# Sliding-window attention in front of two gated feed-forward stages: scores of 64 queries of both heads as one block-diagonal product

## The reference

```
# attention: batch 4, 8 heads, 576 positions, head size 64
scores = q @ k.T / sqrt(64)
scores = where(0 <= i - j < 128, scores - slope[h] * |i - j|, -1e9)
attn   = softmax(scores)           # sum has 1e-9 added
x      = attn @ v                  # heads side by side: 2304 tokens x 512
# first feed-forward stage, inner size 1536
x = (sigmoid(x @ w_gate) * (x @ w_val)) @ w_out
# second stage, inner size 1024
x = ((x @ w1) * (x @ w2)) @ w3 @ w_out2
```

## Time and profile before

| what | us |
|---|---|
| median of 3 timed executions | 923.81 |
| profiled execution, its own time | 921.83 |
| its span | 920.0 |
| PE busy | 891.7 |
| POOL busy | 611.5 |
| DVE busy | 531.9 |
| ACT busy | 487.5 |

### The profile page before, as it was taken

One profiled execution on the slowest core, in us unless ns is written; L12 is line 12 of the kernel. 1 busy time (PEld: TensorE's weight loads), 2 busy tenths in 40 slices (PEclk: granted clock), 3 DMA queues, 4 the chain that ended last, 5 costly groups with the idle time before them and its releaser, 6 DMA issues.

```text
span 920.0 us, 15518 instructions
## 1 busy us (share of the span) xinstructions
PE 891.7 (97%) x5336; PEld 798.6 (87%) x5336; DVE 531.9 (58%) x1235; ACT 487.5 (53%) x1075; POOL 611.5 (66%) x502
## 2 busy tenths in 40 slices
PE   6999999999999999899999999999999999999998
PEld 4666888998988888788898888889999999999997
DVE  5555655565457545555555545755666555575554
ACT  6666585566645644657565654654344333345330
POOL 4449489667654886639956674597769977747930
PEclk9999999999999999999999999999999999999999
DMA  6554423222221222232321322203231221112201
GB/s 227 167 166 137 134 90 109 81 64 74 87 70 61 88 96 88 73 113 95 95 93 44 100 71 67 75 25 92 70 115 68 71 76 66 66 67 70 69 24 69
DMA packets 46142, 80.77 MB, mean 88 GB/s; under 512 B 4208, under 2 KB 27376, under 8 KB 46064
## 3 DMA queue, kind: packets, MB, share of 16 engines
q1 hardware_dynamic: 45648, 79.32, 26.7%
q10 hardware_dynamic: 416, 0.46, 0.1%
HBM read 72.94 MB, written 6.82 MB: 87 GB/s over the span
## 4 chain that ended last, share of the span: by engine, by line
PE 74%; POOL 7%; DVE 6%; issue 5%; ACT 5%; DMA 2%; SPq 0%; ACTq 0%; DVEq 0%; POOLq 0%
PE quad_ps L577 12%; PE quad_ps L579 11%; PE quad_ps L578 11%; PE o_ps L577 10%; PE o_ps L579 9%; PE o_ps L578 9%; PE attn_ps L631 4%; PE attn_ps L599 2%; POOL wo_lo L1223 2%; PE attn_ps L614 2%; PE quad_ps L614 1%; PE quad_ps L599 1%; POOL wq_lo L1210 1%; ACT soft L757 1%; DVE quad_ps L1015 1%
## 5 line engine op out<-in xcount | busy, mean ns | idle before, releaser
L577 PE MATMUL quad_ps<-xs_hi,wq_hi 128*128 128x384 f32 x840 | 292.7, 348 | 4.1 <-POOL wq_lo L1217 2.4
L579 PE MATMUL quad_ps<-xs_hi,wq_lo 128*128 128x384 f32 x840 | 281.6, 335 | 0.0
L578 PE MATMUL quad_ps<-xs_lo,wq_hi 128*128 128x384 f32 x840 | 281.2, 335 | 0.0
L577 PEld LDWEIGHTS quad_ps<-xs_hi,wq_hi 128*128 128x128 f32 x840 | 157.6, 188 | 23.5 <-issue 15.7
L577 PE MATMUL o_ps<-h_hi,wo_hi 128*128 128x384 f32 x480 | 167.1, 348 | 4.5 <-DVE xf L1031 2.3
L579 PE MATMUL o_ps<-h_hi,wo_lo 128*128 128x384 f32 x480 | 161.2, 336 | 0.0
L578 PE MATMUL o_ps<-h_lo,wo_hi 128*128 128x384 f32 x480 | 161.1, 336 | 0.0
L1173 POOL TENSOR_TENSOR soft<-soft,recip 128x512 f32<-128x512 f32 (+2 forms) x80 | 73.6, 920 | 130.6 <-DVE recip L933 130.3
L578 PEld LDWEIGHTS quad_ps<-xs_lo,wq_hi 128*128 128x128 f32 x840 | 157.9, 188 | 0.0
L579 PEld LDWEIGHTS quad_ps<-xs_hi,wq_lo 128*128 128x128 f32 x840 | 157.7, 188 | 0.0
L1210 POOL TENSOR_TENSOR wq_lo<-raw_q,wq_hi 128x768 fp32r<-128x768 f32 x60 | 110.6, 1843 | 68.9 <-ACT wq_hi L791 68.9
(11 more groups left out here) (62 smaller groups left out, 1371.9 us busy)
## 6 DMA issues: line engine op xcount, KB each, us to landing
raw_q<-w SPq DMA_DIRECT2D x24, 512.0 KB, 3.6
raw_q<-w_gate SPq DMA_DIRECT2D x18, 512.0 KB, 3.5
raw_q<-w_val SPq DMA_DIRECT2D x18, 512.0 KB, 4.4
wo_lo_raw<-w_out SPq DMA_DIRECT2D x18, 512.0 KB, 3.6
wo_lo_raw<-w_times_wout SPq DMA_DIRECT2D x12, 512.0 KB, 3.8
w_raw<-w3t SPq DMA_DIRECT2D x16, 256.0 KB, 3.0
outT<-xf SPq DMA_DIRECT2D x8, 384.0 KB, 4.3
q_sb<-qT SPq DMA_DIRECT2D x15, 192.0 KB, 3.9
```

The lines of the kernel that those rows point to most:

```text
L577: pe.matmul(out, lh, rh, start=start, stop=False, skip_group_check=onto)
L578: pe.matmul(out, lh, rl, start=False, stop=False, skip_group_check=onto)
L579: return pe.matmul(out, ll, rh, start=False, stop=stop, skip_group_check=onto)
```

## The change

It touches attention alone. A unit is now 64 queries of both heads. `q_sb` holds, for each unit, a block of 128 rows by 128 columns with the first head's queries in the upper left and the second head's in the lower right; the other two quarters are set to zero once, by six DVE memsets at the start, and the loads write only the blocks: two DMAs for each load of `q`, with pieces of 64 queries (256 bytes). A score matmul takes such a block as weights (128 rows) against all 128 rows of `k_sb`, and gives 128 rows (64 queries of one head above 64 of the other) by 192 keys. A full step has two units and two matmuls of 192 columns; a start step one of 64 and one of 128 columns; a half step one unit, one matmul of 192 columns. `score`, `exponentials` and `normalise` follow this: one instruction per unit of 128 rows by 192 columns (for normalise one for both units). A half step has two transposes instead of four, and `pv` runs over only the queries that are there. Both units' scores lie in one bank. In the head there are two such banks in turn, so `scores(n)` waits for DVE's reading of step n-2. Later `scores` and `pv` share `attn[0]` and `turn` has `attn[1]`: `turn` no longer waits for DVE's reading of the section's scores, `pv` does. In the head `q` and `k` have a third buffer, in memory that is unused until the first feed-forward product P4, and all loads of `q` and `k` are issued one job (in sections: one section) earlier. The bias is half as many rows and 192 columns (96 KB instead of 256 KB).

```diff
@@ sets, buffers
-QC, KC = 3 * P, 4 * P
+KC = 4 * P
+U = P // 2
+UW = WINDOW + U
+QC = 6 * P
...
 def set_of(j):
+    return j % 3 if j < HEAD_JOBS else j % 2
+def v_set(j):
     return j % 2
...
+def units_of(n):
+    return rows_of(n) // U
+def keys_from(n, u):
+    return P - u * U if starts_batch(n) else 0
...
+            q_2, k_2 = sb(early, "q_2", [P, QC // 2], F32), sb(early, "k_2", [P, KC // 2], F32)
...
+        def score_cols(n, u):
+            bank = quad[n % 2] if n < HEAD else attn[0]
+            return bank[:, u * UW + keys_from(n, u):(u + 1) * UW]
         def turn_bank(n):
-            return quad[2 + n % 2] if n < HEAD else attn[0]
-        def pv_bank(n):
-            return attn[n % 2] if n < HEAD else attn[1]
+            return quad[2 + n % 2] if n < HEAD else attn[1]
+        def pv_cols(n):
+            return attn[n % 2][:, 0:rows_of(n)] if n < HEAD else attn[0][:, 2 * UW:2 * UW + rows_of(n)]
+        def q_units(st, h, of, units):
+            return q_sb[st][h * U:(h + 1) * U, 0:units * P].rearrange("p (u h n) -> p u h n", h=2, n=U)[:, :, of, :]
@@ loads
             def load_q(j):
                 wait(sp, qk_done, end_of(before(j)))
-                sp.dma_start(q_sb[set_of(j)][:, 0:m], qT[b * HP + hp, :, q0:q0 + m]).then_inc(q_in[set_of(j)], 16)
+                for h in range(2):
+                    sp.dma_start(q_units(set_of(j), h, h, queries(j) // U), q_from(j, h)).then_inc(q_in[set_of(j)], 16)
...
             load_w3(2)
+            load_k(2)
+            load_q(2)
             load_v(1)
             load_bias(1)
             for s in range(SLOTS + 1):
-                for j in range(2, HEAD_JOBS + 1):
-                    if s == FIRST[j - 1]:
+                for j in range(3, len(JOBS)):
+                    if s == end_of(before(j)) and s <= HEAD:
                         load_k(j)
                         load_q(j)
...
-                    if sec == section_of(j - 1):
+                    if HEAD + sec + 1 == end_of(before(j)):
                         load_k(j)
                         load_q(j)
@@ PE
-                wait(pe, scored, n)
-                if n >= HEAD:
-                    drained = n == HEAD
-                    pe.wait_ge(pt_done, n if drained else n - 1)
-                    pe.wait_ge(x_ready, n if drained else n - 1)
...
+                if n < HEAD:
+                    wait(pe, scored, n - 1)
+                else:
+                    if n > HEAD:
+                        pe.wait_ge(scored, n)
+                    pe.wait_ge(x_ready, n - 1)
...
-                for h in range(2):
-                    rows = slice(h * D, (h + 1) * D)
-                    mm = pe.matmul(score_bank(n, h)[0:m, keys], q_sb[st][rows, q], k_sb[st][rows, where],
-                                   start=True, stop=True)
+                for u in range(units_of(n)):
+                    w = slice((2 * i + u) * P, (2 * i + u + 1) * P)
+                    keys = slice(first + u * U + keys_from(n, u), first + u * U + UW)
+                    mm = pe.matmul(score_cols(n, u), q_sb[st][:, w], k_sb[st][:, keys], start=True, stop=True)
...
             def turn(n):
-                if n < HEAD:
-                    wait(pe, pt_done, n - 1)
+                if n == HEAD:
+                    pe.wait_ge(x_ready, n)
                 else:
-                    wait(pe, scored, min(n + 2, NSTEP))
+                    wait(pe, pt_done, n - 1 if n < HEAD else n)
                 for c in chunks_of(n):
-                    for h in range(2):
+                    for u in range(units_of(n)):
...
             def pv(n):
-                wait(pe, x_ready, n - 1 if n < HEAD else n)
+                if n < HEAD:
+                    wait(pe, x_ready, n - 1)
+                else:
+                    pe.wait_ge(x_ready, n)
+                    pe.wait_ge(scored, min(n + 2, NSTEP))
...
-                        mm = pe.matmul(pv_bank(n)[h * D:(h + 1) * D, 0:P], v_sb[st][rows, left:left + D],
-                                       pt[n % 2][rows, right:right + P], start=c == chunks_of(n)[0], stop=c == 1)
+                        mm = pe.matmul(pv_cols(n)[h * D:(h + 1) * D, :].rearrange("p (u n) -> p u n", n=U),
+                                       v_sb[st][rows, left:left + D], right[:, 0:units, h, :],
+                                       start=c == chunks_of(n)[0], stop=c == 1)
@@ ACT, DVE, POOL
+                if inst == 0 and j == P4:
+                    act.wait_ge(qk_done, HEAD)
...
-                for h in range(2):
+                for u in range(units_of(n)):
                     op = nc.vector.tensor_tensor_reduce(
...
+            for st in range(3):
+                units = (QC if st < 2 else QC // 2) // P
+                nc.vector.memset(q_units(st, 0, 1, units), 0.0)
+                nc.vector.memset(q_units(st, 1, 0, units), 0.0).then_inc(q_zeroed, 1)
...
-                cols = heads(soft[n % 3])[0:rows, :, keys]
+                cols = soft[n % 3][:, :].rearrange("p (u c) -> p u c", u=2)[:, 0:units, lo:UW]
```

More of the change, by code:

```diff
@@ L157, in set_of, with before @@
 def set_of(j):
+    return j % 3 if j < HEAD_JOBS else j % 2
+def v_set(j):
     return j % 2
-def before(j):
-    return max([i for i in range(j) if set_of(i) == set_of(j)], default=None)
+def before(j, of=set_of):
+    return max([i for i in range(j) if of(i) == of(j)], default=None)
 def end_of(j):
@@ L194, in value_loads_to @@
 def value_loads_to(j):
-    return sum(1 + (1 if key_count(i) % P else 0) for i in range(j + 1) if set_of(i) == set_of(j))
+    return sum(1 + (1 if key_count(i) % P else 0) for i in range(j + 1) if v_set(i) == v_set(j))
 def rows_of(n):
@@ L560, in _ @@
                     store_part(g // GP - 1, 3)
-                for u in range(HP + 1, NUNIT):
-                    if sec == section_of(STEP[UNIT_FIRST[u]][0]) - 2:
+                for u in range(HP + 1, NPAIR):
+                    if sec == section_of(STEP[PAIR_FIRST[u]][0]) - 2:
                         load_bias(u)
@@ L751, in exponentials @@
             def exponentials(n):
-                buf, rows = n % 2, rows_of(n)
+                at, units = 2 * (n % 2), units_of(n)
                 act.wait_ge(scored, n + 1)
-                for h in range(2):
-                    cols = heads(soft[n % 3])[0:rows, h, keys_of(n)]
-                    op = nc.scalar.activation(cols, cols, ACT.Exp, scale=-1.0,
-                                              bias=negmax[0:rows, 2 * buf + h:2 * buf + h + 1],
-                                              accum_out=rowsum[0:rows, 2 * buf + h:2 * buf + h + 1])
+                for u in range(units):
+                    op = nc.scalar.activation(soft_cols(n, u), soft_cols(n, u), ACT.Exp, scale=-1.0,
+                                              bias=negmax[:, at + u:at + u + 1],
+                                              accum_out=rowsum[:, at + u:at + u + 1])
                 op.then_inc(exp_done, 1)
@@ L762, in exponentials @@
                 wait(act, recip_done, n - 1)
-                nc.scalar.activation(rowsum2[0:rows, 2 * buf:2 * buf + 2], rowsum[0:rows, 2 * buf:2 * buf + 2],
-                                     ACT.Identity, bias=tiny[0:rows, 0:1]).then_inc(sum_done, 1)
+                nc.scalar.activation(rowsum2[:, at:at + units], rowsum[:, at:at + units],
+                                     ACT.Identity, bias=tiny[:, 0:1]).then_inc(sum_done, 1)
             def out_copy(n):
                 act.wait_ge(pv_done, n + 1)
-                nc.scalar.copy(out_cols(n), pv_bank(n)[:, 0:rows_of(n)]).then_inc(x_ready, 1)
+                nc.scalar.copy(out_cols(n), pv_cols(n)).then_inc(x_ready, 1)
             def turned_copy(n):
@@ L825, in hidden_hi @@
                 nc.scalar.copy(h_hi[g % 2][:, piece(blk)], quad[BANK_OUT[blk]][:, 0:TH]).then_inc(h_hi_done, 1)
-            nc.scalar.dma_start(q_sb[0][:, 0:queries(0)], qT[0, :, 0:queries(0)]).then_inc(q_in[0], 16)
-            nc.scalar.dma_start(heads(bias[0]), bias8[0:2].rearrange("h p c -> p h c")).then_inc(bias_in[0], 16)
+            for h in range(2):
+                nc.scalar.dma_start(q_units(0, h, h, queries(0) // U), q_from(0, h)).then_inc(q_in[0], 16)
+            nc.scalar.dma_start(bias[0][:, :], bias_of[0]).then_inc(bias_in[0], 16)
             act.wait_ge(small_set, 1)
@@ L1330 @@
         "v": np.ascontiguousarray(v.reshape(B, HP, 2, S, D).transpose(0, 1, 3, 2, 4)).reshape(PAIRS, S, P),
-        "bias8": bias,
+        "bias_of": np.ascontiguousarray(bias[:, :U, :UW]).reshape(HP, P, UW),
         "ident": np.eye(P, dtype=np.float32),
```

91 lines of the change are left out of this document (43 added, 48 removed).

## The result

Four executions of the changed kernel took 899.55 to 901.14 us, median 900.19, against a median of 922.93 for the kernel before in runs beside them: ratio 0.9754, 95% interval 0.9742 to 0.9767. The forecast was 909 with a range of 902 to 918. Of the 9.2 us between forecast and median, 7.2 are gain that the sum did not have (21.6 us in the profiled executions). The other 2.0 are the step from the profiled execution to the median, which the forecast took over from the kernel before: here the profiled execution (900.22 us) stands at the median.

What follows compares the result with a forecast made beforehand. PE was taken as the bound. Savings of 7.6 us in sections, 3.6 in slots, 1.2 for k and 2.5 in waits, less 0.5 at the start, took 14.4 from 921.8: 907.4, plus 2.0 for the median, rounded 909; range 902 to 918.

Steps and rivals of the forecast that it cites:

- The full step in sections: Scores of 36 full steps in sections: 0.86 us of PE instead of 0.90; 0.05 less taken each, 1.8 in all.
- start steps: Eight start steps in sections: the 0.09 us of entry go, records stay bound by loads; 0.8 us less in all.
- The columns: Scores on PE: the half-zero full-array product costs almost the same as paired heads, which overlap in one record of four.
- Half steps: Eight half steps in sections: scores 0.22 us less, transposes 0.20, pv 0.20; together 5.0 us less.
- Slots: Stretch from 10 to 103 us: full steps 0.6 us more, half steps 4.2 less; 3.6 us less work on PE.
- The k wait: PE's one wait for late k goes with a third buffer and a load one job earlier: 1.2 us less.
- Waits: PE's waits for DVE's scores and POOL's normalise and weight splits, 6.8 us: 2.5 counted as gained.
- The start: Small q pieces while DMA engines are full delay w3's second piece and folds: 0.5 us more taken.
- (a): Rival: saved PE time returns as waits for POOL and DVE; half the gain stays, 7.2 us, 916.6; chance 0.18.
- (b): Rival: the start's delay is paid in full, 3.3 us instead of 0.5, giving 912; chance 0.11.
- (c): Rival: float32 weight loads of full-array scores can't hide behind running matmuls; 27 us more, 936; chance 0.07.
- (d): Rival: half steps' pv and transposes set by something other than columns; only 10 us gained; no chance of its own.

Runs made afterwards that it cites:

- v first: Changed kernel with v's load issued ahead of k's and q's in the slots: 899.88 us, ratio 0.9746, beside the changed kernel's 901.86.
- pv of half steps: Changed kernel with half steps' pv on the full array, both heads' v as 128 weight columns: 899.65 us, ratio 0.9747.
- the tiled scores: Changed kernel with each block's score product made as two 64-row matmuls, one per head: 916.24 us, ratio 0.9940.

## Why the prediction was right in kind and too small

**PE is the bound, and its work decides.** Right: PE's share stayed at 97%, and of the 16.1 us in sections 14.0 are passages and 1.7 waits of PE.

**The full step in sections.** This is the step that failed. I wrote "0.17 + 4 x 0.173 = 0.86; on leaving, some 0.01 us less. I take 0.05 less each". It saves 0.18. In the prediction's own terms, up to the first product behind, the passage was to take 0.86 us after 0.90 and took 0.69. Two things were mis-sized. The records cost 0.160 us, not 0.173; I had taken the spacing of the products, whose 0.013 is paid once for a passage and not for each record. And leaving the form of 64 rows costs 0.1 us as entering does, where the sum had 0.01. I had seen the next products 0.28 us apart behind scores and 0.26 apart behind transposes, which never leave the full form, and took that for the same cost of any passage. Behind transposes it fits a start of the product that is stamped early: 0.36 us from the first of four to the product, where their columns and loads last 0.43. Read to the second product, transposes have no exit cost and scores had one. With 36 full steps that is 4.7 us more; start steps (0.17 instead of 0.10) and half steps (0.77 in all their passages instead of 0.62) give another 1.8.

**The columns.** Right: full-array scores stream as long as the tiled ones did, 4 x 0.160 against 3 x 0.213, which is what records of two tiles that go in order would give. The order itself was not varied. The 2x that the Trainium skill, TensorEngine Tiling (Array Packing), Theoretical Speedup, gives as the most from row tiles isn't reached here: both heads' product took 0.64 us in tiles and takes 0.64 on the full array, half of it zeros.

**Half steps.** Two transposes save 0.22 (0.20 forecast). pv over 64 columns saves 0.21; the 0.20 of the forecast was a choice between 0.27 and nothing, so that it fits is in part luck.

**Slots.** 5.0 us for 4.8 forecast, and the agreement is luck in part. PE's waits in the slots fell only from 1.8 to 1.1 us, as three for v came for the one for k that went; the work between them is 4.3 us shorter for 3.6 forecast. And in the profiles of the kernels whose slots have the same work for PE the slots took 86.9 to 90.5 us, and what differs is chiefly the waits for loads (for v none to 2.6 us). The forecast named the second q DMA on SP and called it free in sections; it did not price it in the slots, where v's load stands behind it (v first: 1.5 us less there). The k wait went as said.

**Waits.** 1.7 us gained for 2.5 forecast in the profiled stretch. What "is late next" was named rightly: DVE's additions and POOL's splits.

**The start.** 0.9 us later for 0.5 forecast, but in the profiles of the other kernels that load q in pieces the first fold lies between 9.95 and 11.7 us, and there is one profile of before (9.97), so its size isn't settled. The path was another than the forecast's, which had the second piece of w3 as what is late: the first scores started at 7.5 us instead of 4.2, and the first fold waited for DVE's work behind them. In 1 to 5 us the q pieces took 19 ns each, near the lower of my two bounds (13 and 53); from the DMA view of this stretch (packets, MB, share):

```profile
q10 hardware_dynamic: 714, 0.18, 21.6%
```

**The rivals.** The saved time as waits (a) did not happen for this change, as PE's waits in sections fell; it is what befell pv of half steps, and the same give and take shows in part in the tiled scores. The start in full (b), 3.3 us, did not come: 0.9, and 1.8 at most in the profiles of the variants. The unhidden float32 loads (c) did not come: the scores' records are 0.160 us apart, which is their columns' time, and leave no room for a load of 0.105 in line. The sentence in the Trainium skill, TensorE: Matmul & The Clock Gate, The mechanism, that loads overlap running matmuls only when the row group differs is contradicted here for float32 as well; the same section also names a background weight buffer, which would allow what the trace shows. (d) did not come either: both terms of the half steps saved what was forecast.

**The end.** 1.2 us that nobody forecast: the last matmul is followed by 4.45 us before and by 3.3 us in the profiles of the changed kernel and its variants. The trace of before has one instruction packet (16 KB, 1.3 us) among the last DMAs, that of after none in this stretch. That it is the cause was not tried.

## What to carry to other kernels

Price a passage of PE from the last matmul before it to the second one behind it; the start of the first one behind comes too early to show an exit cost. Where small matmuls of another tile form stand between full-array ones, count 0.2 us or more for each in-and-out beside their columns; a full-array product that computes twice as much, half of it zeros, can be the cheaper one. Once a saving of PE is in, look at the next engine's time in the same section before the next edit: here 2.2 us less of PE's work gave nothing.

## What was not expected of the hardware

- Entering and leaving the form of 64 rows around a matmul of 64 columns cost 0.34 us more than the same matmul with 128 rows, for half the arithmetic. Around a group of scores the same cost 0.19 us.
- Two row tiles whose float32 matmuls are issued one head after the other take the time of three records for four, 0.64 us for 256 columns, and of five for eight, 1.00 us with drains for 192 columns.
- SP needs 0.61 us (median) to issue a DMA for q in pieces of 256 bytes, against 0.43 us for one in rows, and 1.27 us for the two of a load; four loads in the slots took 1.7 to 2.3 us.
